# Routing logits from 64-row matmuls, shared zeroing, more transposes ahead of the attention loop, and one fold turn in the next stage

## The reference, cut to what matters

```python
# attention: B,H,S,D = 4,8,768,48, a decayed state per head
for t in range(S):
    cur = einsum('bhd,bhe->bhde', u*k[t], v[t])
    y[t] = einsum('bhd,bhde->bhe', r[t], state + cur)
    state = w * state + einsum('bhd,bhe->bhde', k[t], v[t])
x = y as (B*S, H*D) = (3072, 384)
# routing and 8 experts, F = 1024
keep = x @ w_skip > 0
logits = x @ w_gate                      # 8 columns
e, gate = argmax and its softmax weight
x[keep] += gate * (relu(x @ w1[e]) @ w2[e])
# two gated layers
out = (((x @ m1) * (x @ m2)) @ w3) @ w_out   # w3 @ w_out is folded into one matrix first
```

## Time and profile before

| | us |
|---|---|
| median of 3 runs (673.34 to 675.14) | 675.08 |
| the profiled execution, its own time | 678.15 |
| its span, first to last instruction | 676.4 |
| attention (until the last copy on ACT) | 0 to 148.4 |
| routing | 148.7 to 189.9 |
| experts, gated layers | 190.2 to 676.4 |

### The profile page before, as it was taken

The page is one execution under the profiler, slowest core; times in us unless marked ns, Lnnn a source line. Parts: engine busy times, 40 slices in busy tenths (PEclk is TensorE's granted clock), DMA queues, the critical chain, the costliest instruction groups (busy, mean ns, idle before and its releaser), DMA issues. The chain is left out here.

```text
span 676.4 us, 17764 instructions
## 1 busy us (share of the span) xinstructions
PE 638.2 (94%) x7532; PEld 574.5 (85%) x7532; DVE 298.0 (44%) x445; ACT 215.9 (32%) x374; POOL 168.0 (25%) x185
## 2 busy tenths in 40 slices
PE   6799999999999897997898999999999999999997
PEld 6799999965689896996896888888888888888886
DVE  6356676519356677675741223223223223223222
ACT  1134333422445454553433213213213212222222
POOL 6456766513533343433313100000000000000000
PEclk8879999999999898998999999999999999999999
DMA  8558889737136756176304002002002001001001
GB/s 134 104 105 167 164 167 181 225 97 293 32 128 247 242 201 246 69 239 242 116 30 147 1 0 88 7 0 76 19 0 72 23 1 48 0 1 47 0 1 47
DMA packets 104088, 67.76 MB, mean 100 GB/s; under 512 B 79490, under 2 KB 98084, under 8 KB 104048
## 3 DMA queue, kind: packets, MB, share of 16 engines
q1 hardware_dynamic: 75824, 57.88, 29.5%
q10 hardware_dynamic: 26176, 4.74, 3.8%
q0 software_dynamic: 2048, 4.58, 2.0%
HBM read 56.31 MB, written 12.58 MB: 102 GB/s over the span
## 5 line engine op out<-in xcount | busy, mean ns | idle before, releaser
L1369 DVE TENSOR_TENSOR gl_g_sb<-gl_a_sb,gl_pab 128x512 f32<-128x512 f32 x48 | 33.0, 688 | 186.3 <-ACT gl_a_sb L1346 186.3
L1289 PE MATMUL gl_pab<-gl_xT_hi,wm_lo 128*128 128x512 f32 x288 | 112.9, 392 | 0.0
L1289 PE MATMUL gl_pab<-gl_xT_lo,wm_hi 128*128 128x512 f32 x288 | 112.8, 392 | 0.0
L1289 PE MATMUL gl_pab<-gl_xT_hi,wm_hi 128*128 128x512 f32 x288 | 112.2, 389 | 0.0
L1346 ACT ACTIVATE gl_a_sb<-gl_pab 128x512 f32<-128x512 f32 x48 | 28.7, 597 | 184.0 <-PE gl_pab L1289 184.0
L1304 PE MATMUL gl_po<-gl_wf_hi,gl_g_hi 128*128 128x384 f32 x192 | 65.6, 342 | 0.7 <-DVE gl_g_lo L1371 0.7
L1304 PE MATMUL gl_po<-gl_wf_hi,gl_g_lo 128*128 128x384 f32 x192 | 64.8, 337 | 0.0
L1304 PE MATMUL gl_po<-gl_wf_lo,gl_g_hi 128*128 128x384 f32 x192 | 64.6, 336 | 0.0
L1289 PEld LDWEIGHTS gl_pab<-gl_xT_hi,wm_lo 128*128 128x128 f32 x288 | 54.0, 188 | 11.3
L1289 PEld LDWEIGHTS gl_pab<-gl_xT_lo,wm_hi 128*128 128x128 f32 x288 | 54.1, 188 | 10.4
L1289 PEld LDWEIGHTS gl_pab<-gl_xT_hi,wm_hi 128*128 128x128 f32 x288 | 54.1, 188 | 10.3
(11 more groups left out here) (197 smaller groups left out, 1293.4 us busy)
## 6 DMA issues: line engine op xcount, KB each, us to landing
ew_w_in<-in_moe_w SPq DMA_DIRECT2D x16, 1536.0 KB, 7.0
w_in<-in_moe_w SPq DMA_DIRECT2D x14, 512.0 KB, 7.2
k_in<-in_k SPq DMA_DIRECT2D x48, 96.0 KB, 3.8
r_in<-in_r SPq DMA_DIRECT2D x48, 96.0 KB, 3.3
v_in<-in_v ACTq DMA_DIRECT2D x48, 96.0 KB, 3.6
xbuf<-x_nat SPq DMA_DIRECT2D x24, 192.0 KB
gl_x_in<-xbuf SPq DMA_DIRECT2D x12, 384.0 KB, 4.4
out<-gl_o_sb SPq DMA_DIRECT2D x12, 384.0 KB, 2.5
```

The lines of the kernel that those rows point to most:

```text
L1289: m = pe.matmul(p_ab[f % 2][w][:, :], a[:, w * KD + k, cols], b[t.slot][:, k, :], start=(k == 0 and n == 0), stop=(k == KD - 1 and n == 2))
L1369: dve.tensor_tensor(g_sb[f % 2][:, :], a_sb[f % 2][:, :], p_ab[f % 2][1][:, :], ALU.mult).then_inc(s_g, 1)
```

## The change

In attention, `logits` is split over the two halves of rows: for each q and each cg, a matmul with 64 rows of `YT` and 64 rows of `w_gates`, into bank cg of `p_Y`, at a place that depends on the slot alone. The two half sums of a chunk are copied out by ACT once a chunk (`logits_out`, ahead of `y_out` of slot 0, and once after the last turn), and DVE adds them into `lg` at the end. Three of the zeroed pieces go from DVE to POOL and `v_bonus[0]` is zeroed only in its 16 padding columns. After each of the two transposes groups of `k_rev`, PE does 8 transposes more. `turn(1)` and `turned(1)` move from the end of attention to the beginning of routing, and `product(1)` is cut in two halves around the rank matmuls.

```diff
             def logits(t):
                 for q in range(HP):
-                    i = pe.matmul(p_Y[:, 0, bass.ds(t.num(NL, LG0), NL)], YT[t.pr][:, q % 2, (q // 2) * P:(q // 2 + 1) * P], w_gates[:, q, :],
-                                  start=(q == 0), stop=(q == HP - 1), skip_group_check=True)
+                    for cg in range(2):
+                        i = pe.matmul(p_Y[:, cg, HALF + t.slot * NL:HALF + (t.slot + 1) * NL], YT[t.pr][half(cg), q % 2, (q // 2) * P:(q // 2 + 1) * P],
+                                      w_gates[half(cg), q, :], start=(q == 0), stop=(q == HP - 1), skip_group_check=True)
...
                 i.then_inc(s_kpT, 1)
-            pe.wait_ge(s_pad, 3)
-            pe.wait_ge(s_zero, 11)
+                keep_warm(pe, ident, p_R[:, 0, :], 8)
+            pe.wait_ge(s_pad, 6)
+            pe.wait_ge(s_zero, 8)
...
                 if f is logits and at(c, j, NT + 1):
-                    fold.turn(pe, 1, [p_R[:, i, :] for i in range(2)])
                     fold.product(pe, 0, p_AU[:, 0, :])
...
+            def logits_out(c):
+                return act.activation(lg_parts[:, bass.ds(c * LW, LW)].rearrange("p (g x) -> p g x", g=2), p_Y[:, :, HALF:HALF + LW // 2], ACT.Copy)
+
             def y_out(t):
                 wait(act, s_Y, t.done())
+                if t.slot == 0 and not at(t.c, t.j, 0):
+                    logits_out(t.c - 1)
                 act.activation(YT[t.pr][:, :, :], p_Y[:, :, 0:HALF], ACT.Copy).then_inc(s_YT, 1)
...
                 if f is y_out and at(c, j, NT):
-                    fold.turned(act, 1, [p_R[:, i, :] for i in range(2)])
+                    act.wait_ge(s_Y, BASE + NT + 1)
+                    logits_out(NCH - 1).then_inc(s_lg, 1)
                     fold.taken(act, 0, p_AU[:, 0, :])
...
-            for x in (w_gates[:, :, :], state[0][:, :, :, :], state[1][:, :, :, :], v_bonus[0][:, :, :], v_bonus[1][:, :, :], YT[0][:, :, :], YT[1][:, :, :],
-                      A_m[1][:, :, :, :], rT[1][:, :, :, :], k_dec[:, NS - 1, :, 0:D], v_in[:, NS - 1, :, 0:D]):
+            for x in (w_gates[:, :, :], v_bonus[0][:, :, D:DP], state[0][:, :, :, :], state[1][:, :, :, :],
+                      YT[0][:, :, :], YT[1][:, :, :], A_m[1][:, :, :, :], rT[1][:, :, :, :]):
                 dve.memset(x, 0.0).then_inc(s_zero, 1)
...
-            dve.wait_ge(s_Y, BASE + NT + 1)
-            dve.tensor_copy(lg[:, :, :], p_Y[:, 0, LG0:LG0 + NT * NL].rearrange("p (n e) -> p e n", e=NL))
+            dve.wait_ge(s_lg, 1)
+            parts = lg_parts[:, :].rearrange("p (c g s e) -> p g e c s", c=NCH, g=2, s=NS)
+            dve.tensor_tensor(lg[:, :, :].rearrange("p e (c s) -> p e c s", s=NS), parts[:, 0], parts[:, 1], ALU.add)
...
                 pool.memset(x[:, :, :, D:DP], 0.0).then_inc(s_pad, 1)
+            for x in (v_bonus[1][:, :, :], k_dec[:, NS - 1, :, 0:D], v_in[:, NS - 1, :, 0:D]):
+                pool.memset(x, 0.0).then_inc(s_pad, 1)
...
-                fold.product(pe, 1, p_W[1])
+                fold.turn(pe, 1, p_T[1])
+                fold.product(pe, 1, p_W[1], (0, 1))
...
                 pe.matmul(p_tot, ones[:, :], m16, start=True, stop=True).then_inc(s_mm, 1)
+                fold.product(pe, 1, p_W[1], (2, 3))
...
             def _(act):
+                fold.turned(act, 1, p_T[1])
                 act.wait_ge(s_exp, 1)
```

More of the change, by code:

```diff
@@ L128, in attention @@
         HALF = HP * C
-        LG0 = HALF + 2 * NL
+        LW = 2 * NS * NL
         r_in = sb("r_in", [P, NS, H, DP])
@@ L145, in attention @@
         state_sum = [sb(f"state_sum{i}", [P, 2, HP, D]) for i in range(2)]
+        lg_parts = sb("lg_parts", [P, NCH * LW])
         w_sq = sb("w_sq", [P, 8, HP])
@@ L170, in attention @@
         s_scaled = [sem(f"s_scaled{i}") for i in range(2)]
-        s_zero = sem("s_zero")
+        s_zero, s_lg = sem("s_zero"), sem("s_lg")
         BASE = 4
@@ L562, in values @@
                                    bonus[t.pr][:, :].unsqueeze(2).broadcast_to([P, H, D]), ALU.mult).then_inc(s_vb, 1)
-            pool.wait_ge(s_zero, 5)
+            pool.wait_ge(s_zero, 2)
             schedule(pool, ((products, 2), (new_state, -1), (values, 1)), 2, 0)
```

## The result

The changed kernel takes **707.61 us** (median of four executions) against 675.11 us of the kernel before in the same session: slower, and outside the predicted range. The ratio is 1.0286 (95% interval 1.023 to 1.0341). The ratio compares the lower group alone, so that it is the smaller of the two losses; the profiled execution is one of the upper, 721.05 us with a span of 719.3.

A forecast was written before the change was run, and what follows sets the result against it. PE's own instruction stream was taken to bound the kernel (busy 638.2 of 676.4 us). Terms of -1.5, -1.0, -2.4 and +1.6 gave -3.3, so 671.8 us; range 667.5 to 679, the forecast's own 668.5 to 675.5.

The forecast's parts named there:

- the loop's code no longer stays: Attention loop: entering the eighth block fetches a ninth, the loop's first is lost; 692 to 710 us, or 729; chance 0.14.
- each block pushes out the next one: Attention loop, within the 0.14 rival: every pass costs what the first does, +11.5, 729 us.
- Ahead of the loop: Before attention's loop: zeroing moved and idle transposes added let the loop start 1.5 us earlier, at 10.9 (bounds 1.0 and 1.7).
- The clock at the start: PE nearly gapless from 7.6 us, so full clock where it was half from 10.65 to 20.89; no half clock before 40.
- the third rival: Start and first pass: added transposes at half clock, loop starts 1 us later, 675.8 us; with a near case, chance 0.21.
- The first pass: Attention loop's first pass goes at the code fetch's pace: 29.2 us against 30.15, -1.0 (-2.7 to +0.9).
- Logits: Attention turns: halves load side by side, a change of shape goes; 0.11 us in 22 turns, -2.4 us (-1.1 to -4.4).
- Copies of the logits: ACT in attention: `YT` delayed some 0.25 us in one turn in four, covered, so 0; uncovered 1.5 us.
- The fold turn: Attention loses `turn(1)`, -0.85; routing gains 2.47 as PE waits for ACT's copies; net +1.6 us (+1.2 to +2.5).
- The sum: Whole kernel: -1.5 - 1.0 - 2.4 + 1.6 = -3.3 us, put on the median of 675.08, gives 671.8 us.

The follow-up runs named there:

- the old loop pushed down: The kernel before with 70 instead of 24 idle transposes at the very start, its loop ending 21 instructions into the eighth block: 723.3 us, ratio 1.0723.
- the new one moved to the next block: The changed kernel with 67 instead of 24 idle transposes at the start, its loop lying in the second to the eighth block: 674.09 us, ratio 0.9977.
- all six points of the table: The changed kernel (24) and it with 13, 16, 32, 44 or 64 first idle transposes, 0 to 101 instructions in the eighth block: medians 671.14 to 766.37 us.

## Why the prediction was wrong

**The step that failed** is the one on which the forecast stood without a term of its own: that the loop's code stays after its first pass though the pass "enters the eighth" block. The rival that says otherwise, "the loop's code no longer stays", is what happened, and I gave it 0.14. In place of a loop whose code stays the runs showed two events in the profiled execution, each a stop of 5.8 us and a pass 12.4 us longer, 36.4 us where the sum had nothing. The trace of before had all of its premises: blocks of 256, eight seen and none more, 21 instructions in the eighth. Against it I had only that no block was seen fetched twice, which a loop of seven blocks could not show. Shown by the runs is that, for loops of this length, position alone decides (the old loop pushed down is slow, the new one moved to the next block or cut to end before the eighth is not), and that an event is nine fetches. The Trainium skill, page "Advanced Engine Details and Errata", section ISA Cache, gives TensorE 128 KB and a line of 16 KB, 256 instructions; worked out from these figures, an estimate, that is room for eight. The traces agree with eight: in all nine kernels whose loop lies in seven blocks these stay, though one block more is fetched beside them (in eight of the nine: six fetches in the first pass, and by the prediction's count two blocks there at the start).

That a block is fetched before PE enters it is shown by the kernel moved to the next block: its loop lies in the second to the eighth, and at the end of its first pass a ninth is fetched (the seventh fetch, at 42.49 us). If that pushes out the first, it is one that the loop does not need, and indeed nothing is fetched again. How an event runs I read from the order of the fetches, which is argued and not shown by a run of its own: some 1.3 us after the branch back out of the eighth block a fetch begins (79.16), and a second right behind it (79.70), a ninth block and then the loop's first, pushed out by it; from there each fetch pushes out the block that is wanted next, so that the whole pass is fetched again. That is the rival's harder variant, "each block pushes out the next one", +11.5 a pass; measured are 30.6 - 18.2 = 12.4 for the pass and 5.8 for the stop, 18.2 an event, and 2.3 to 3.7 more in a pass where the clock is down behind it. With one event a time of 693 to 696 is within the rival's 692 to 710, with two it lies between that and its 729. That is luck: the rival had one wait in each of five passes or a whole refetch in each, and neither happened. What I had not seen is that it doesn't come at every branch back: 0 to 5 of five. After a pass that was fetched again the next branch has none, except with 101 instructions in the eighth block. A likely reason, not shown, is that the eighth block has only just come and PE leaves it at once; more instructions in it make an event likelier. That the time spent in the eighth block decides fits all six points of the table, but what exactly sends out the request is open.

**Ahead of the loop**: right. Start at 10.91 us (predicted 10.9).

**The clock at the start**: wrong. It held from 7.8 to 18.0, but not, as I expected, through the first 40 us: PE waited 2.04 us for code until 16.79 and 2.27 until 38.54, and each of the two long stretches at half clock begins within 1.3 us of such a wait. The transposes did keep the clock full before 18 us: 0.90 for a run of 8 (predicted 0.8). By the Trainium skill, page "TensorE: Matmul & The Clock Gate", Part 4, the full rate does not engage for transposes; the trace disagrees, since PE had done nothing but transposes when the clock rose at 7.8 us, and a run took 0.90 us at the full clock and 1.72 at half (the idle runs on the kernel before). With 13 first idle transposes the first added run took 1.72 us as well, and the loop still started at 12.33 us, 0.1 earlier than before and not 1 later as the third rival had it.

**The first pass**: 28.54 us against 29.2 predicted (10.91 to 39.45), within the bounds. That the clock is "mostly not paid out" was too strong: first passes lasted 26.1 to 30.3 us over the seven-block kernels, and those with at most 10.2 us of half clock in the first 60 us took 26.2 to 28.0, the kernel before 30.15 with 17.1. The tie is loose: the second trace of the logits split took 26.1 with 13.7.

**Logits**: right in mechanism. The halves load side by side (16 loads in 0.99 us), and the change of shape on entry costs 0.17 us less, of which I had taken 0.11. Steady passes of 18.35 us without the idle runs, against 18.67, give 0.08 a turn, -1.8 us in 22 turns against -2.4. The 7.8 us measured for the edit alone are more than this: of the 8.2 by which its two spans are shorter than the two of before, 2.4 lie in the first pass and 4.6 in the experts, where the sum had nothing, and only 1.0 in the steady passes.

**Copies of the logits**: as taken. `logits_out` takes 0.23 us (69.04 in the changed kernel), and without the idle runs PE waits for `YT` once, 0.3 us.

**The fold turn**: the step was right in its parts: in routing, from the first load to `turn(2)`, 7.96 us with it and 5.46 without (predicted 8.08 and 5.61), on the changed kernel without the idle runs; on the kernel before, with the clock at half, it was 9.03. Routing as a whole is 2.8 us longer with it by the same two traces, and 4.1 in the changed kernel's (predicted 2.5). The sum of +1.6 lies in both intervals, +0.7 (-0.9 to +2.4) on the kernel before and +4.0 (some 1 to 7) on the changed one; neither pins it down further.

**The sum**: -3.3 was worth having where its condition held. With 13 instead of 24 idle transposes, everything else as in the change, the kernel takes 671.14 us, where the forecast said 671.8. That is luck of the terms: its ratio of 0.9917 is -5.6 us in its own session, not -3.3, and in its trace, 9.0 us shorter than the one before, hardly a term has its size: -0.1 ahead of the loop (predicted -1.5), -3.9 in the first pass (-1.0), -2.5 in the rest of attention (-3.2 with `turn(1)` gone), +3.0 in routing (+2.5), -6.0 in the experts and +0.5 in the gated layers (nothing in either).

## What to carry to other kernels

Where a loop's code fills nearly all the blocks that an engine keeps, count in instructions where its first and last lie in the stream, edits ahead of the loop included: 16 idle transposes cost 24 or 49 us here, and 11 fewer in another place gave it all back. A limit that the old kernel never crossed leaves no mark in its trace, so "never seen" is no evidence against it; give such a rival the chance that its premises have. And a profile in which the instruction queue fetches in the steady part of a loop has the first explanation of idle "issue" time to look at there.

## What the runs showed of the hardware that I had not expected

- Being over the edge is not all or nothing: 5, 21, 37, 61 and 101 instructions in the eighth block gave 0 or 1, 1 or 2, 2, 2 and 5 refetched passes, and single times of one program up to 28 us apart (693 and 721).
- One fetch too many costs nine: in the changed kernel a branch back that finds its block gone stops PE for 5.8 us, and the pass behind it takes 12.4 us longer.
- Kernels that differ only ahead of the experts spend 159.2 us (the one with 67 idle transposes) to 167.1 (before) in them, and the waits for gathered rows that I summed range from 9.7 to 14.7 us.
- Time at half clock differs between executions of one program too: of the first 60 us it was 23.9 in one trace of the logits split and 13.7 in the other, and 3.4 in the kernel with 67 idle transposes. In the experts 3.4 to 17.1 us of it go with the length of the stage.
